# Head of token mixing: tile turns ahead of the angle products, and angle products amid the token products

## The chip, the core and the metric

The kernel runs on one core of one Trainium2 chip. The metric is the device time of one execution in microseconds (us). Shapes are fixed; all inputs and outputs are 32-bit floats. The core has five engines that run at the same time and wait for each other through semaphores: PE (TensorE, matrix products and transposes), DVE (VectorE), ACT (ScalarE), POOL (GpSimd), and SP, which here only issues DMA transfers.

## The reference, cut to what matters

```python
# attention: B=4, H=8, S=768, D=64, 4 sink keys and a window of 128
scores = where(keep, q @ k.T * scale, -1e9);  a = softmax(scores)
x = (a @ v), heads side by side                     # (B, S, 512)

# token mixing
theta = x @ w_theta                                 # (B, S, 512)
zr, zi = x * cos(theta), x * sin(theta)
y = einsum('ts,bsd->btd', w_tok_r, zr) + einsum('ts,bsd->btd', w_tok_i, zi)
u = x + y
x = u + maximum(u @ w_ch, 0)                        # channel mixing

# gated part
gate = sigmoid(causal depthwise conv of x, 5 taps)
out = (gate * (x @ w_val)) @ w_out
```

## The kernel before

The program has three stages, one behind the other on every engine: attention over 16 pairs of heads (a loop written out by hand per engine), token mixing over 4 batches, channel mixing and the gated part over 8 half batches.

Token mixing takes a batch in six tiles of 128 tokens. The fp32 products are made of three passes with a high and a low part of each operand (`split_passes`). For tile s of batch b the work is a chain through all engines:

- `turn` (PE, L1463): four transposes of the tile `x_nat` into the bank `ps_x`.
- `xT` (ACT L1163, L1165; DVE L1295): a raw copy of the turned tile (stored to `xT_scratch` by SP), its high part `xT_hi` and its low part `xT_lo`.
- `theta` (PE, L1474): 12 matmuls of 512 columns into the bank `ps_th`: the angles. There is one bank, so the next `theta` waits for `r_part_done`.
- `turns_out` (DVE L1302, L1305, L1307): rounds the angle to whole turns (`k_big`, `k_int`) and takes them off (`r_part`, which has the place of `k_big`, and in the profile its name). `angle` (DVE L1313, L1317, L1321): `r_raw`, `r_in`, `r_abs`.
- `sines` (ACT L1171, L1173) and `z_parts` (DVE L1330, ACT L1181, POOL L1104): z = x sin and x cos, `z_raw`, with high part `z_hi` and low part `z_lo`.
- `tokens` (PE, L1485): 48 matmuls per tile, into six banks `acc`, one block of banks j = 0 to 5 after the other (6 matmuls of 512 columns each for j < 4, 12 of 256 columns each for j = 4 and 5). At the first tile of a batch each block waits for `u_done`, the addition (DVE L1353, `add_x`) that empties its bank of the batch before.

The loop over tiles (`token_body`) puts on PE at step s: `theta` of the tile two ahead, `turn` of the tile three ahead, then all of `tokens(b, s)`. At the last step of the last batch it puts `first_channels` (PE L1534, channel products) ahead of `tokens`. They wait for `uT_lo` (POOL L1120, `lo_u`), which comes behind the last `z_lo` on POOL, and for the split of the channel weights (`split_w3`: ACT L1192, DVE L1343), which comes behind the last z on ACT and DVE.

The head is the place where attention ends and token mixing begins. There the order is written out by hand on each engine (L368 to L380 for ACT, L454 to L475 for DVE, L581 to L603 for PE), with the last pieces of attention between the first pieces of mixing: `pv` (PE L540, a product with v into `ps_y`), `evac_y` (the copy of `ps_y` into `y_sb`, DVE L409 or ACT L350), `turn_y` (PE L554 and L556, into `ps_o`), and `normalise` (DVE L426, `ps_o` into `x_sb`, counted by `normed`). The banks `acc` lie over those of attention, so PE waits for the last `normalise` before the token products (L602).

Of the kernel before, what the change touches and what calls it, by code (L numbers as in the profile page):

```python
# [21 lines left out]
ACT = mybir.ActivationFunctionType  # L22

P = 128
B, H, S, D = 4, 8, 768, 64
C = H * D
T = S // P
# [4 lines left out]
PAIRS = B * H // 2  # L32
# [22 lines left out]

SyncMix = namedtuple("SyncMix", "begin store_xT run")
PoolMix = namedtuple("PoolMix", "constants chain run")
ScalarMix = namedtuple("ScalarMix", "begin xT sines z_parts run")
VectorMix = namedtuple("VectorMix", "begin xT turns_out angle z_parts run")
TensorMix = namedtuple("TensorMix", "begin turn theta run")  # L60
Mixing = namedtuple("Mixing", "sync gpsimd scalar vector tensor")
# [7 lines left out]
def wait_count(eng, sem, count):  # L69

    if isinstance(count, int) and count <= 0:
        return
    eng.wait_ge(sem, count)
# [21 lines left out]
def fast_path(nc, early, qT, kT, vP, vS, w2, x_scr, xT_scr, uT_scr, w2h, w2l, ident, x_nat, x_in, w3, w3h, w3l, uT0,  # L95
# [6 lines left out]
    IT = PAIRS // 2  # L102
    VISITS = T // 2
# [6 lines left out]
    with ExitStack() as ctx:  # L110
# [37 lines left out]
        y_sb = [place(nc, f"y_sb{m}", [P, 2 * P], F32, U_SB_AT + 8 * P * m) for m in range(VISITS)]  # L148
# [166 lines left out]
        @block.scalar  # L315
        def _(act):
            def exp(n, s, v, t, e):
                g = SCORES * n + 4 * v + 2 * t + e
                k = VISITS * n + v
                i = 2 * v + t  # L320
                lo, hi = columns(i)
                act.wait_ge(maxed, g + 1)
                if t == 0:
                    wait_count(act, turned, 2 * (k - 3) + e + 1)
                    wait_count(act, gathered, 2 * (n - 1) + e + 1)
                nc.scalar.activation(probs[e][:, i, lo:hi], masked[2 * t + e][:, lo:hi], ACT.Exp,  # L326
                                     bias=neg_max[:, s, e, i:i + 1], scale=-1.0,
                                     accum_out=row_sum[:, s, e, i:i + 1]).then_inc(exped, 1)

            def evac(k, m):  # L330

                act.wait_ge(turned, 2 * k + 2)
                wait_count(act, pv_done, k - 2)
                if m > 0:
                    nc.scalar.copy(probsT[1][:, 2 * m:2 * m + 2, :], ps_t[1][:]).then_inc(evac_a, 1)
                else:
                    nc.scalar.copy(probsT[1][:, 0:2, :].rearrange("p t k -> p (t k)")[:, P:4 * P],
                                   ps_t[1][:].rearrange("p t k -> p (t k)")[:, P:4 * P]).then_inc(evac_a, 1)

            def evac_sinks(n):  # L340

                act.wait_ge(turned, 2 * VISITS * (n + 1) + 2)
                wait_count(act, y_turned, VISITS * n)
                nc.scalar.copy(sinkT[:], ps_t[1][:, 0, 0:P]).then_inc(sink_evac, 1)

            def evac_y(n):

                act.wait_ge(pv_done, VISITS * n + 2)
                wait_count(act, y_turned, VISITS * (n - 1) + 2)
                nc.scalar.copy(y_sb[1][:], ps_y[:, 0:2 * P]).then_inc(y_evac[1], 1)  # L350

            def step(it, first=False):
                for s in range(2):
                    n = 2 * it + s
                    for v in range(VISITS):
                        k = VISITS * n + v
                        for t in range(2):
                            for e in range(2):
                                exp(n, s, v, t, e)
                        if v == 1 and not (first and s == 0):  # L360
                            evac_y(n - 1)
                        if not (first and s == 0 and v == 0):
                            evac(k - 1, (v - 1) % VISITS)
                        if v == 1 and not (first and s == 0):
                            evac_sinks(n - 1)

            step(0, first=True)
            with act.Fori(1, IT) as it:  # L368
                step(it)
            mix = mixes.scalar(act)  # L370
            mix.xT(0, 0)
            evac(VISITS * PAIRS - 1, VISITS - 1)
            evac_y(PAIRS - 1)
            evac_sinks(PAIRS - 1)
            mix.xT(0, 1)
            mix.sines(0, 0)
            mix.xT(0, 2)
            mix.z_parts(0, 0)
            mix.sines(0, 1)
            mix.z_parts(0, 1)  # L380
            mix.run()

        @block.vector
        def _(dve):
# [77 lines left out]

            dve.wait_ge(exped, SCORES * PAIRS)
            dve.wait_ge(v_ready, PAIRS)
            mix.turns_out(0, 0)
            evac_y(PAIRS - 1, 2)
            mix.xT(0, 1)
            mix.angle(0, 0)
            normalise(PAIRS - 1, 1, IT - 1, False)
            mix.turns_out(0, 1)  # L470
            mix.xT(0, 2)
            mix.z_parts(0, 0)
            mix.angle(0, 1)
            mix.z_parts(0, 1)
            mix.run()  # L475
# [2 lines left out]
        def _(pe):  # L478
# [112 lines left out]
            turn_y(PAIRS - 1, 1, 0)  # L591
            pe.wait_ge(w_lo_done, B * H)
            pe.wait_ge(maxed, SCORES * PAIRS)
            mix.theta(0, 0)
            mix.turn(0, 1)
            pv(PAIRS - 1, 1, 2, IT)
            turn_y(PAIRS - 1, 1, 1)
            turn_y(PAIRS - 1, 1, 2)
            mix.theta(0, 1)
            mix.turn(0, 2)  # L600

            pe.wait_ge(normed, 2 * PAIRS)  # L602
            mix.run()  # L603
# [217 lines left out]
def mixing(nc, ctx, tag, x_scr, xT_scr, uT_scr, w2h, w2l, ident, x_nat, x_in, w3, w3h, w3l, uT0, conv, out):  # L821
# [336 lines left out]
    def scalar(act):  # L1158
# [104 lines left out]
                    gates(*nxt, 2)  # L1263
                    gates(*nxt, 3)

        def first_sines(b, s):
            act.wait_ge(const2, 1)
            sines(b, s)

        def begin():  # L1270
            xT(0, 0)
            xT(0, 1)
            first_sines(0, 0)
            z_parts(0, 0)
            xT(0, 2)
            chain(0, 1)
# [8 lines left out]
                gates(0, 0, k)  # L1285
            channel_batches(act, channel_body)

        return ScalarMix(begin, xT, first_sines, z_parts, run)

    def vector(dve):  # L1290
        def xT(b, s):
# [165 lines left out]
    def tensor(pe):  # L1457
# [28 lines left out]
                                            stop=s == T - 1 and m == 1 and a == 2, skip_group_check=True)  # L1486
            return last

        def tokens(b, s):

            pe.wait_ge(z_lo_done, 2 * (T * b + s) + 2)
            for j in range(T):
                if s == 0:
                    pe.wait_ge(u_done, T * b + j + 1)
                if j < CB:
                    last = block_of(s, j, acc[j][:], slice(0, C), True)
                else:
                    for h in range(2):
                        last = block_of(s, 2 * (j - CB) + h, acc[j][:, h * (S - C):(h + 1) * (S - C)],
                                        slice(C, S), h == 0)  # L1500

                if s == T - 1:
                    last.then_inc(acc_done, 1)
                elif j == T - 1:
                    last.then_inc(tok_done, 1)

        def token_body(b, last):
            for s in range(T):
                if s < T - 2:
                    theta(b, s + 2)  # L1510
                elif not last:
                    theta(b + 1, s + 2 - T)
                if s < T - 3:
                    turn(b, s + 3)
                elif not last:
                    turn(b + 1, s + 3 - T)
                if last and s == T - 1:
                    first_channels()
                tokens(b, s)

        def first_channels():

# [251 lines left out]
```

## Time and profile before

| | us |
|---|---|
| median of 3 runs | 663.4 (662.34 to 663.86) |
| profiled execution | 665.1 |
| span of its profile | 663.3 |
| attention, up to the head | 0 to about 170 |
| head, up to the first token product | about 170 to 187.7 |
| token mixing | 187.7 to about 470 |
| channel mixing and gate | from 446.9 to the end |

The chain of waits (which work released which, followed back from the last instruction) and the list of waits tell where PE stood. Matmuls are pipelined: a group's start in the timeline can lie a tenth or two before the time at which the chain of waits puts it, and an instruction's own duration (0.39 us for one of 512 columns) is longer than the distance to the next (0.23 us). In the window table a row is: stretch, length, then the busy time of each engine with its count, the granted clock of PE as a share of full speed, the DMA share and GB/s.

### The profile page before, as it was taken

What the parts mean: (1) busy time and instruction counts of PE and PEld (TensorE: products, weight loads), DVE (VectorE), ACT (ScalarE), POOL (GpSimd) and SP (SyncE); (2) the same over time, 40 slices, a digit from 0 to 9 for tenths busy, and PEclk for the clock granted to TensorE, in tenths of its full rate; (3) what the DMA queues carried; (4) which work ended last, traced back from release to release, by engine and by line L of the source; (5) the groups of instructions that cost most, each with busy time, mean ns of one, the idle gap of its engine ahead of it and who ended that gap; (6) DMA issues with size and microseconds to landing.
All of it is one profiled execution on the core that took longest, in us unless ns stands there. A gap on an engine that the chain in (4) does not pass through costs nothing.

```text
span 663.3 us, 14158 instructions
## 1 busy us (share of the span) xinstructions
PE 643.6 (97%) x4016; PEld 549.8 (83%) x4016; DVE 419.3 (63%) x1008; ACT 294.7 (44%) x775; POOL 253.4 (38%) x323
## 2 busy tenths in 40 slices
PE   6899999999889999999999999999999999999995
PEld 4677777777778888888888888889999999999994
DVE  4588788778775446463564547778768458458450
ACT  4777777777542322422232323443243243243231
POOL 4455465565142211313131221346355345345320
PEclk9799999999999999999999999999999999999999
DMA  7376666764512135222432237330520220220011
GB/s 247 132 225 203 240 215 208 243 210 164 176 48 65 33 95 161 60 63 79 133 104 60 82 94 240 103 122 1 190 96 30 67 95 28 69 95 26 23 48 52
DMA packets 61048, 76.70 MB, mean 116 GB/s; under 512 B 4176, under 2 KB 41040, under 8 KB 61008
## 3 DMA queue, kind: packets, MB, share of 16 engines
q1 hardware_dynamic: 61008, 76.24, 35.6%
q8 instruction: 16, 0.26, 0.2%
q14 instruction: 24, 0.20, 0.1%
HBM read 51.06 MB, written 25.17 MB: 115 GB/s over the span
## 4 chain that ended last, share of the span: by engine, by line
PE 92%; issue 2%; POOL 2%; DMA 1%; SPq 1%; DVE 1%; ACT 0%; POOLq 0%; DVEq 0%; ACTq 0%
PE acc L1485 30%; PE ps_p L1534 18%; PE ps_o L1574 10%; PE ps_th L1474 10%; PE ps_s L491 7%; PE ps_t L517 7%; PE ps_y L540 7%; PE ps_o L554 2%; PE ps_x L1463 1%; DMA v_sink<-vS 1%; DMA x_res<-xT_scratch 1%; PE ps_o L556 1%; POOL g_lo L1136 0%; POOL z_lo L1104 0%; SPq L1716 0%
## 5 line engine op out<-in xcount | busy, mean ns | idle before, releaser
L1104 POOL TENSOR_TENSOR z_lo<-z_raw,z_hi 128x512 fp32r<-128x512 f32 x48 | 62.5, 1323 | 206.4 <-ACT z_hi L1181 206.4
L1485 PE MATMUL acc<-w2h,z_hi 128*128 128x512 f32 (+1 forms) x384 | 131.2, 342 | 0.9 <-POOL z_lo L1104 0.9
L1485 PE MATMUL acc<-w2l,z_hi 128*128 128x512 f32 (+1 forms) x384 | 129.3, 337 | 0.0
L1485 PE MATMUL acc<-w2h,z_lo 128*128 128x512 f32 (+1 forms) x384 | 129.3, 337 | 0.0
L326 ACT ACTIVATE probs<-masked,neg_max 128x260 f32<-128x260 f32 (+1 forms) x192 | 92.5, 483 | 37.9 <-DVE neg_max L393 25.5
L393 DVE CUSTOM_DVE_ANT_0 masked<-ps_s,mask 128x260 f32<-128x260 f32 (+1 forms) x192 | 69.0, 403 | 39.1 <-PE ps_s L491 32.5
L1485 PEld LDWEIGHTS acc<-w2h,z_hi 128*128 128x128 f32 x384 | 72.8, 190 | 9.0 <-issue 1.2
L1485 PEld LDWEIGHTS acc<-w2h,z_lo 128*128 128x128 f32 x384 | 72.8, 190 | 8.0
L1485 PEld LDWEIGHTS acc<-w2l,z_hi 128*128 128x128 f32 x384 | 72.9, 190 | 7.8
L1295 DVE TENSOR_TENSOR xT_lo<-ps_x,xT_hi 128x512 fp32r<-128x512 f32 x24 | 16.6, 690 | 78.2 <-ACT xT_hi L1165 78.2
L1398 DVE SCALAR_TENSOR_TENSOR ps_g<-m_raw,conv_w,ps_g 128x384 f32<-128x384 f32 x112 | 62.0, 617 | 0.2
L491 PE MATMUL ps_s<-k_sb,q_sb 64*128 64x260 f32 (+1 forms) x384 | 55.2, 404 | 5.1 <-DMA k_sb<-kT 5.1
L1136 POOL TENSOR_TENSOR g_lo<-g_raw,g_hi 128x384 fp32r<-128x384 f32 x32 | 32.5, 1015 | 71.4 <-ACT g_hi L1237 71.4
L1171 ACT ACTIVATE sin_cos<-r_in 128x512 f32<-128x512 f32 x24 | 15.2, 633 | 97.3 <-DVE r_in L1317 97.3
L517 PE MATMUL ps_t<-ident,probs 128*128 128x128 f32 x352 | 51.5, 283 | 2.1 <-ACT probs L326 2.1
L540 PEld LDWEIGHTS ps_y<-probsT,v_sb 128*64 128x64 f32 x512 | 30.7, 138 | 23.1 <-issue 16.3
L1437 DVE TENSOR_TENSOR g_raw<-ps_p,gate 128x384 f32<-128x384 f32 x32 | 17.8, 557 | 50.7 <-PE ps_p L1534 50.6
L540 PE MATMUL ps_y<-probsT,v_sb 128*64 128x128 f32 (+1 forms) x512 | 49.7, 326 | 0.0
L1128 POOL TENSOR_TENSOR m_lo<-m_raw,m_hi 128x384 fp32r<-128x384 f32 x32 | 33.5, 1046 | 39.8 <-ACT m_hi L1224 39.8
L517 PEld LDWEIGHTS ps_t<-ident,probs 128*128 128x128 f32 x352 | 38.8, 143 | 11.2 <-issue 7.9
L1534 PE MATMUL ps_p<-uT_hi,w_hi 128*128 128x384 f32 x128 | 42.9, 335 | 0.9 <-DVE m_raw L1382 0.9
L491 PEld LDWEIGHTS ps_s<-k_sb,q_sb 64*128 64x128 f32 x384 | 33.1, 194 | 12.9 <-issue 8.4
(93 smaller groups left out, 1435.8 us busy)
## 6 DMA issues: line engine op xcount, KB each, us to landing
k_sb<-kT SPq DMA_DIRECT2D x16, 396.0 KB, 3.9
q_sb<-qT SPq DMA_DIRECT2D x16, 384.0 KB, 3.2
v_sb<-vP SPq DMA_DIRECT2D x16, 384.0 KB, 4.5
x_scratch<-x_sb SPq DMA_DIRECT2D x16, 384.0 KB, 2.6
x_nat<-x_scratch SPq DMA_DIRECT2D x24, 256.0 KB, 3.0
xT_scratch<-xT_raw SPq DMA_DIRECT2D x24, 256.0 KB, 2.2
x_res<-xT_scratch SPq DMA_DIRECT2D x24, 256.0 KB, 3.2
uT_scratch<-u_sb SPq DMA_DIRECT2D x24, 256.0 KB, 2.6
```

The costliest lines, as they stand in the source:

```text
L326: nc.scalar.activation(probs[e][:, i, lo:hi], masked[2 * t + e][:, lo:hi], ACT.Exp, bias=neg_max[:, s, e, i:i + 1], scale=-1.0, accum_out= ...
L393: nc.vector.tensor_tensor_reduce(masked[2 * t + e][:, lo:hi], ps_s[e][t][:, lo:hi], m[:], -SCALE, 3.0e38, ALU.add, ALU.min, neg_max[:, s, ...
L491: nc.tensor.matmul(ps_s[e][t][:, lo:hi], q_sb[s][rows, i * P:(i + 1) * P], k_sb[s][rows, first:first + hi - lo], start=True, stop=True).th ...
L517: last = nc.tensor.transpose(ps_t[e][:, t, side * P:(side + 1) * P], probs[e][:, i, at:at + P], ident[:])
L540: last = nc.tensor.matmul(ps_y[rows, dst:dst + width], v_sb[s][:, j, rows], keysT, start=a == 0, stop=a == len(passes) - 1, skip_group_che ...
L1104: nc.gpsimd.tensor_tensor(z_lo[s % ZR][:, part, :], z_raw[:, part, :], z_hi[s % ZR][:, part, :].bitcast(F32), ALU.subtract).then_inc(z_lo_ ...
L1128: nc.gpsimd.tensor_tensor(m_lo[:, k, :], m_raw[c][:, k, HALO:HALO + L], m_hi[:, k, :].bitcast(F32), ALU.subtract).then_inc(m_lo_done, 1)
L1398: nc.vector.scalar_tensor_tensor(out=summed, in0=src, scalar=w, in1=summed, op0=ALU.mult, op1=ALU.add).then_inc(tap_done[k], 1)
L1474: last = nc.tensor.matmul(ps_th[:], l, r, start=k == 0 and a == 0, stop=k == CB - 1 and a == 2)
L1485: last = nc.tensor.matmul(bank, l, r, start=first and s == 0 and m == 0 and a == 0, stop=s == T - 1 and m == 1 and a == 2, skip_group_chec ...
L1534: last = nc.tensor.matmul(bank[:, 0:L], l, r, start=kk == 0 and a == 0, stop=kk == CB - 1 and a == 2)
L1574: last = nc.tensor.matmul(bank[:], l, r, start=kk == 0 and a == 0, stop=kk == CB - 1 and a == 2)
```

## The change

Four moves, all in order; no product and no transfer is added or dropped, and one small activation is new.

1. PE's head: `turn(0, 1)` now comes ahead of `theta(0, 0)`, and `turn(0, 2)` ahead of `theta(0, 1)`.
2. PE's loop: at each step but a batch's last, blocks 0 to 2 of `tokens` come first, then `theta` and `turn`, then blocks 3 to 5. At the last step all of `tokens` comes behind them, as before.
3. ACT's head: a sine of one column (`sine_table`) brings the sine table in early; the copy `evac_y` of the last `ps_y` moves from DVE to ACT; `xT(0, 2)` comes ahead of the first sines.
4. DVE's head: `xT(0, 1)` ahead of the first rounding, the first angle and z of tile 0 ahead of the second rounding, and the last `normalise` behind the second rounding.

```diff
@@ ScalarE, end of attention
             mix.xT(0, 0)
             evac(VISITS * PAIRS - 1, VISITS - 1)
-            evac_y(PAIRS - 1)
+            evac_y(PAIRS - 1, 1)
             evac_sinks(PAIRS - 1)
             mix.xT(0, 1)
+            mix.sine_table()
+            evac_y(PAIRS - 1, 2)
+            mix.xT(0, 2)
             mix.sines(0, 0)
-            mix.xT(0, 2)
             mix.z_parts(0, 0)
@@ VectorE, end of attention
+            mix.xT(0, 1)
             mix.turns_out(0, 0)
-            evac_y(PAIRS - 1, 2)
-            mix.xT(0, 1)
             mix.angle(0, 0)
-            normalise(PAIRS - 1, 1, IT - 1, False)
-            mix.turns_out(0, 1)
             mix.xT(0, 2)
             mix.z_parts(0, 0)
+            mix.turns_out(0, 1)
+            normalise(PAIRS - 1, 1, IT - 1, False)
             mix.angle(0, 1)
@@ TensorE, end of attention
+            mix.turn(0, 1)
             mix.theta(0, 0)
-            mix.turn(0, 1)
             pv(PAIRS - 1, 1, 2, IT)
             turn_y(PAIRS - 1, 1, 1)
             turn_y(PAIRS - 1, 1, 2)
+            mix.turn(0, 2)
             mix.theta(0, 1)
-            mix.turn(0, 2)
@@ ScalarE, mixing
-        def first_sines(b, s):
+        def sine_table():
+
             act.wait_ge(const2, 1)
-            sines(b, s)
+            nc.scalar.activation(sin_cos[:, 0, 0:1], half_pi[:], ACT.Sin)
@@ TensorE, mixing
-        def tokens(b, s):
-
-            pe.wait_ge(z_lo_done, 2 * (T * b + s) + 2)
-            for j in range(T):
+        def tokens(b, s, banks_of_step):
+
+            if 0 in banks_of_step:
+                pe.wait_ge(z_lo_done, 2 * (T * b + s) + 2)
+            for j in banks_of_step:
@@
         def token_body(b, last):
             for s in range(T):
+
+                ahead_of = 0 if s == T - 1 else T // 2
+                tokens(b, s, range(0, ahead_of))
                 if s < T - 2:
                     theta(b, s + 2)
@@
                 if last and s == T - 1:
                     first_channels()
-                tokens(b, s)
+                tokens(b, s, range(ahead_of, T))
```

How the instructions stand now, at three places. First PE where the head passes into the loop over batches. `ps_th` is a product of `theta`, `ps_x` the four transposes of `turn`; the branch and what is beside it open the loop. Before:

```order
L1474 MATMUL ps_th<-w2l,xT_hi_155 128x512
L1474 MATMUL ps_th<-w2h,xT_lo_157 128x512
L1463 MATMUL ps_x<-ident,x_nat_56 128x128 x4
L951 UNCONDITIONAL_BRANCH
L951 ISA
L73 REGISTER_ALU
L1474 MATMUL ps_th<-w2h,xT_hi_154 128x512
```

and now:

```order
L1477 MATMUL ps_th<-w2l,xT_hi_155 128x512
L1477 MATMUL ps_th<-w2h,xT_lo_157 128x512
L952 UNCONDITIONAL_BRANCH
L952 ISA
L1498 REGISTER_ALU
L1488 MATMUL acc<-w2h,z_hi_158 128x512
L1488 MATMUL acc<-w2l,z_hi_158 128x512
```

The angle product of tile 2 and the turn of tile 3 no longer stand between the head and the first token product.

Second, DVE in the head, from the last `normalise` (`x_sb`) or the angle of tile 0 (`r_abs`) on. Before:

```order
L426 TENSOR_TENSOR x_sb_144<-ps_o,inv_sum 128x512
L1302 TENSOR_SCALAR k_big<-ps_th 128x512
L1305 TENSOR_SCALAR k_int<-k_big 128x512
L1307 SCALAR_TENSOR_TENSOR k_big<-k_int,ps_th 128x512
L1295 TENSOR_TENSOR xT_lo_156<-ps_x,xT_hi_154 128x512
L1330 TENSOR_TENSOR z_raw<-x_nat_54,sin_cos 128x512
L1330 TENSOR_TENSOR z_raw<-x_nat_54,sin_cos 128x512
```

and now:

```order
L1324 SCALAR_TENSOR_TENSOR r_abs<-r_in 128x512
L1298 TENSOR_TENSOR xT_lo_156<-ps_x,xT_hi_154 128x512
L1333 TENSOR_TENSOR z_raw<-x_nat_54,sin_cos 128x512
L1333 TENSOR_TENSOR z_raw<-x_nat_54,sin_cos 128x512
L1305 TENSOR_SCALAR k_big<-ps_th 128x512
L1308 TENSOR_SCALAR k_int<-k_big 128x512
L1310 SCALAR_TENSOR_TENSOR k_big<-k_int,ps_th 128x512
L428 TENSOR_TENSOR x_sb_144<-ps_o,inv_sum 128x512
```

The two products of z stood behind the second rounding and now stand ahead of it; the last `normalise` went from the front of this piece to its end.

Third, PE in the last batch, where the last angle product (`theta` of tile 5) begins. Before, behind the end of the token products of tile 2:

```order
L1485 MATMUL acc<-w2h,z_hi_160 128x256
L1485 MATMUL acc<-w2l,z_hi_160 128x256
L1485 MATMUL acc<-w2h,z_lo_163 128x256
L1474 MATMUL ps_th<-w2h,xT_hi_155 128x512
L1474 MATMUL ps_th<-w2l,xT_hi_155 128x512
```

and now, behind the first three blocks of tile 3:

```order
L1488 MATMUL acc<-w2h,z_hi_158 128x512
L1488 MATMUL acc<-w2l,z_hi_158 128x512
L1488 MATMUL acc<-w2h,z_lo_161 128x512
L1477 MATMUL ps_th<-w2h,xT_hi_155 128x512
L1477 MATMUL ps_th<-w2l,xT_hi_155 128x512
```

It begins 18 token matmuls later than before; the `first_channels` products stand where they stood.

## Rows read from the trace of the kernel before

**Rows 1.** The page: busy time, share and instructions of each engine.

```profile
PE 643.6 (97%) x4016; PEld 549.8 (83%) x4016; DVE 419.3 (63%) x1008; ACT 294.7 (44%) x775; POOL 253.4 (38%) x323
```

**Rows 2.** Who PE waited for, 160 to 250 us: total, times, longest.

```profile
PE ps_th L1474 <- DVE xT_lo L1295: 2.2, 1, 2.2
PE acc L1485 <- POOL z_lo L1104: 0.9, 1, 0.9
```

**Rows 3.** Timeline of the head: start, duration, engine, line, [idle before].

```profile
174.81 0.69 DVE L1302 TENSOR_SCALAR k_big<-ps_th 128x512 f32<-128x512 f32 x1 [2.42 <-PE ps_th L1474]
...
175.04 1.09 PE L540 MATMUL ps_y<-probsT,v_sb 128*64 128x256 f32 x12
175.14 0.59 ACT L1163 COPY xT_raw<-ps_x 128x512 f32<-128x512 f32 x1 [3.11 <-PE ps_x L1463]
...
175.62 0.59 ACT L1165 CAST xT_hi<-ps_x 128x512 fp32r<-128x512 f32 x1
...
176.59 0.42 DVE L409 COPY y_sb<-ps_y 128x256 f32<-128x256 f32 x1
...
177.07 0.33 PE L554 MATMUL ps_o<-ident,y_sb 128*128 128x128 f32 x1 [0.43 <-DVE y_sb L409]
...
178.75 1.28 ACT L1171 ACT_TABLE_LOAD   x1 [2.53 <-DVE r_in L1317]
...
179.31 0.69 DVE L426 TENSOR_TENSOR x_sb<-ps_o,inv_sum 128x512 f32<-128x512 f32 x1
...
183.14 1.28 DVE L1330 TENSOR_TENSOR z_raw<-x_nat,sin_cos 128x512 f32<-128x512 f32 x2
...
183.36 0.49 PE L1474 MATMUL ps_th<-w2h,xT_hi 128*128 128x512 f32 x1 [2.21 <-DVE xT_lo L1295]
...
184.56 3.03 POOL L1104 TENSOR_TENSOR z_lo<-z_raw,z_hi 128x512 fp32r<-128x512 f32 x2 [15.49 <-ACT z_hi L1181]
...
185.06 1.40 DVE L1317 TENSOR_SCALAR r_in<-r_raw 128x512 f32<-128x512 f32 x1
```

**Rows 4.** The chain of waits, head and first steps: start, duration, what.

```profile
171.93 2.76 PE ps_th L1474 x12
...
187.72 8.62 PE acc L1485 x48
...
199.09 0.44 PE ps_x L1463 x4
```

**Rows 5.** Instructions of two tiles: duration ns min/median/max, first and last start.

```profile
L1305 DVE TENSOR_SCALAR k_int<-k_big x24: 426/428/428, 175.5 to 431.0; 128x512 f32<-128x512 f32 x24
...
L1104 POOL TENSOR_TENSOR z_lo<-z_raw,z_hi x48: 1284/1291/1822, 184.6 to 436.7; 128x512 fp32r<-128x512 f32 x48
```

**Rows 6.** Last batch: timeline of DVE and POOL, then the chain of waits.

```profile
430.24 0.69 DVE L1302 TENSOR_SCALAR k_big<-ps_th 128x512 f32<-128x512 f32 x1 [0.55 <-PE ps_th L1474]
...
438.22 5.51 POOL L1120 TENSOR_TENSOR uT_lo<-uT,uT_hi 128x384 fp32r<-128x384 f32 x4
...
446.85 8.32 PE ps_p L1534 x48
```

**Rows 7.** End of batch 0: the chain of waits, then the timeline of DVE.

```profile
245.74 8.38 PE acc L1485 x48
...
247.57 0.68 DVE L1302 TENSOR_SCALAR k_big<-ps_th 128x512 f32<-128x512 f32 x1
...
250.66 0.69 DVE L1321 SCALAR_TENSOR_TENSOR r_abs<-r_in 128x512 f32<-128x512 f32 x1
...
252.78 1.88 DVE L1353 TENSOR_TENSOR u_sb<-acc,x_res 128x512 f32<-128x512 f32 x3
```

**Rows 8.** A stall in attention, then table of stretches (the granted clock follows POOL).

```profile
18.86 0.66 PE L517 MATMUL ps_t<-ident,probs 128*128 128x128 f32 x3 [2.09 <-ACT probs L326]
...
19.00:26.00 7.00, 6.65 (x33) 4.44 (x33) 4.01 (x19) 5.64 (x22) 4.09 (x9) 0.51 0.20 54
180.00:184.00 4.00, 1.79 (x11) 1.29 (x10) 3.19 (x6) 2.39 (x6) 0.00 (x0) 1.00 0.54 164
```

More of the change, by code:

```diff
@@ L57 @@
 PoolMix = namedtuple("PoolMix", "constants chain run")
-ScalarMix = namedtuple("ScalarMix", "begin xT sines z_parts run")
+ScalarMix = namedtuple("ScalarMix", "begin sine_table xT sines z_parts run")
 VectorMix = namedtuple("VectorMix", "begin xT turns_out angle z_parts run")
@@ L344, in evac_sinks, with evac_y @@
                 nc.scalar.copy(sinkT[:], ps_t[1][:, 0, 0:P]).then_inc(sink_evac, 1)
[L346 to L350, printed above, removed]
+            def evac_y(n, m):
+                act.wait_ge(pv_done, VISITS * n + m + 1)
+                wait_count(act, y_turned, VISITS * (n - 1) + m + 1)
+                nc.scalar.copy(y_sb[m][:], ps_y[:, 0:2 * P]).then_inc(y_evac[m], 1)
             def step(it, first=False):
@@ L360, in step @@
                         if v == 1 and not (first and s == 0):
-                            evac_y(n - 1)
+                            evac_y(n - 1, 1)
                         if not (first and s == 0 and v == 0):
@@ L1264, in channel_body @@
                     gates(*nxt, 3)
-        def first_sines(b, s):
+        def sine_table():
             act.wait_ge(const2, 1)
-            sines(b, s)
+            nc.scalar.activation(sin_cos[:, 0, 0:1], half_pi[:], ACT.Sin)
         def begin():
+            sine_table()
             xT(0, 0)
             xT(0, 1)
-            first_sines(0, 0)
+            sines(0, 0)
             z_parts(0, 0)
@@ L1286, in run @@
             channel_batches(act, channel_body)
-        return ScalarMix(begin, xT, first_sines, z_parts, run)
+        return ScalarMix(begin, sine_table, xT, sines, z_parts, run)
     def vector(dve):
```

## The prediction, made before the changed kernel was run

> **What bounds the kernel now.** I read the page's busy times first: PE is busy for 97% of the span [rows 1], so only PE's idle time and its clock can be won or lost. Then the list of PE's waits around the head [rows 2]: 2.2 us before the angle product of tile 2, for `xT_lo`, and 0.9 us before the first token product, for `z_lo`. The timeline adds 0.43 us for the copy `y_sb` on DVE (the row at 177.07 [rows 3]). Together about 3.5 us, and the whole gain of the head cannot exceed that. From 187.72 us on the chain of waits is PE alone, step after step, of which rows 4 show the pieces: there a reordering gives nothing unless it makes PE wait.
>
> **Part 1, the head, walked through.** The question is when the first token product starts. Before, it started at 187.72 with one `theta` (2.75) and one `turn` (0.44) already done [rows 4]. Now these 3.19 us come after it. So the new order breaks even if token products start at 187.72 - 3.19 = 184.53.
> - PE: `turn(0, 1)` takes its 0.44 first, so `theta(0, 0)` starts at 171.93 + 0.44 = 172.37 and ends at 175.13 [rows 4]; `pv` still starts at 175.04 or a tenth later and ends at about 176.15 [rows 3]. DVE's first `k_big` moves from 174.81 to 175.25, as much later as `theta`.
> - ACT: the raw copy and `xT_hi` end 1.1 us behind the turn (turn's end at about 175.1, `xT_hi` at 176.21 [rows 3]), so `xT(0, 1)` ends near 173.5, the table load takes 1.28 [rows 3], the sine of one column an estimated 0.2: done by 175.0, which is before `pv` ends. So the load costs nothing here. If it ran late by more than 1.1 us, it would delay the copy. The copy itself (0.42 on DVE [rows 3], taken as the same on ACT) ends at 176.6 instead of 177.0, since DVE no longer does the rounding first; PE's 0.43 us stall goes.
> - `turn(0, 2)` starts at about 177.2, so `xT_hi` ends near 178.9. DVE has meanwhile run the rounding and the angle of tile 0 without a break. Undisturbed, `r_abs` ends 3.78 us behind the start of `k_big` (250.66 + 0.69 less 247.57 [rows 7]): at 179.0, with `r_in` at 178.3. ACT does the sine (0.63 by an estimate from the copies' 0.59, the cosine a little more) behind `xT_hi`, until 180.1; DVE does `xT_lo` (0.69) in between, and `z_raw` (1.28 [rows 3]) runs from 179.65 to 180.95. Before, it ran from 183.14 [rows 3].
> - POOL started `z_lo` 1.42 us behind the first `z_raw` (184.56 less 183.14 [rows 3]): now at 181.0. Two of them took 3.03 us there while DVE's `r_in` was stretched to 1.40 [rows 3], and take 2 x 1.29 when undisturbed [rows 5]. They end at 183.6 to 184.1.
> - But DVE has `k_big`, `k_int`, `r_part` and the last `normalise` still to do, and PE waits for that too. `k_big` starts at 180.9, `k_int` would start at 181.6, while the first `z_lo` runs. `k_int` was never disturbed before (428 ns at most [rows 5]); `r_in`, the same kind of operation, ended at 186.46, which is 0.6 us behind the end of the first `z_lo` (184.56 + 1.29). I take that: `k_int` ends at 182.9, `r_part` (0.69) at 183.6, `normalise` (0.69 [rows 3]) at 184.25, and the token products start at 184.35.
>
> The Trainium skill, "SBUF — State Buffer", section "SBUF: two separate sides", says that VectorE and GpSimd share one pair of ports as an exclusive lock, which a VectorE operation wants only in a two-port mode or with two inputs in SBUF. By that `k_int` is blocked, and `r_part` and `normalise` with one input in PSUM are not, which is the sum above; without the lock it would be 183.7.
>
> So the head gains 184.53 - 184.35 = 0.2 us; between -0.6 (if `r_part` and `normalise` are held up by the second `z_lo` as well, 0.8 us) and +0.85 (if nothing is). PE's three short stalls become one of 3.6 us. It begins with the end of `theta(0, 1)`: before, PE fell idle at 183.36 - 2.21 = 181.15 [rows 3], behind `theta` and a `turn` of 0.44; now the `turn` is done earlier and the idle time begins at 180.7.
>
> **Part 2, the loop.** At each step but the last, `theta` and `turn` come 18 matmuls of 0.23 us later (12 took 2.75 [rows 4]): 4.1 us. Their consumers follow 4.1 us later. In the middle of a batch nobody is near. From the end of a `theta` to the token products of its tile PE has 0.4 + 4.3 us of its own step and 11.6 of the next one: 16.3. The chain needs 3.8 for the rounding and the angle [rows 7], 4.5 from `z_raw` to the end of `z_lo` (183.14 to 187.59 [rows 3]) and an estimated 2 for the `xT` ahead of it: some 10.5, so 5 us are left.
> - At a batch's end, step 5 keeps its order, but the tokens of the next batch follow at once, without 3.2 us of `theta` and `turn` between. They need `u_sb` of bank 0. It starts at 252.78 and takes 0.69, and ACT's later z delays it by an estimated 0.25: 253.7. PE needs it at 245.74 + 8.38 = 254.12 [rows 7]. The margin is 0.4 us; the next blocks have more. Cost zero, and at most an estimated 0.5 us for each of three batch ends if it is missed.
> - In the last batch the last `theta` is 4.1 us later, so is `k_big` (it waited for just that, 0.55 idle [rows 6]), and all that follows it: z, the weight splits, and on POOL `uT_lo`, which is queued behind the last `z_lo`. It ended at 438.22 + 5.51 = 443.73; it will end at 447.85. PE wants it for `first_channels` at 446.85 [rows 6]. With 0.1 us for the semaphore that is a new stall of 1.1 us, and behind it stand all later products. Bounds: 0.3 to 1.6, from errors of half a microsecond in the shift. The end of the stage hangs on PE's products, so nothing later gives it back.
>
> **Part 3, the clock.** In attention PE stood idle for 2.09 us up to 18.86, and from 19 to 26 us the granted clock was 0.51 in the mean, that is 1.2 GHz instead of 2.4 for about 6.8 of the 7 us [rows 8]. The stall of 2.21 us in the head left the clock at 1.00 (180 to 184 [rows 8]). So a stall of 2 us can do either. The new one of 3.6 us is longer than both. If the clock falls, PE's dense token products run at half speed for as long as it lasts. At 6.8 us that costs 3.4 us; at nothing, 0. What ran in the slow stretch of rows 8 had gaps and small matmuls; the token products are dense, so I take the middle, 1.7 us.
>
> The Trainium skill, "TensorE: Matmul & The Clock Gate", Part 1, names the half rate the default and says that activity releases it. By that rule gathering two short pauses into one long one is what this change should not do; rows 8 show one case for it and one against.
>
> **The sum.** Without the clock: -0.2 + 1.1 = +0.9 us. With it: -0.2 + 1.1 + 1.7 = +2.6 us. On the profiled execution (span 663.3, with 1.8 us around it 665.1) that is 667.7; on the median of 663.4 it is 666.0.
>
> **The rivals.**
> - A, *the clock falls in the head* (forecast), 666.0: for it, the length of the stall; against it, the 2.21 us stall that did nothing.
> - B, *the clock stays*: 663.4 + 0.9 = 664.3, which is no change that can be told. It holds if the pause is not long enough, or if `z_lo` and `normalise` come earlier than I have them.
> - C, *not slower*: `uT_lo` is in time. Its four pieces take 5.51 us [rows 6] while DVE splits weights beside them; in another alignment they may need 4.4, and the stall of 1.1 us is gone. Then -0.2 gives 663.2, and with an undisturbed `k_int` as well -0.85 gives 662.5. The point from which it decides is a `uT_lo` that ends before 446.8.
> - D, *the batch ends*: `u_sb` of bank 0 is later than PE, at three places, by up to 0.5 us each: +0.9 + 1.5 = 665.8, more with the clock. For it: only 0.4 us of margin; against it: the addition of bank 0 waited for nothing but DVE's own chain, which moves with PE.
> - That the change does not do what it says: the order of instructions shows that it does.
>
> **How the numbers follow.** A has 0.46, B 0.30, C 0.12, D 0.12. The forecast is A's 666.0. B and C reach down to 662.5, A with its full price of 3.4 to 667.7. The range of 662.9 to 667.4 leaves out the ends of C and the dearest part of A, some 2 in 10. Less than 0.2% (1.3 us, so 662.1 to 664.7) can hardly be told from no change. Slower by more: most of A (0.38), a quarter of B (0.07), most of D (0.09), together 0.54. Faster by more: only the far end of C and a head better than all my bounds, 0.06. The rest, 0.40, is no change.
>
> **What the changed profile would show.** Right: PE's 0.43 and 2.2 us waits gone, one wait of about 3.6 us before the first `acc` product, put down to `x_sb` or `z_lo`; the table load ahead of the copy of `ps_y` on ACT; `k_int` of tile 1 stretched to over 1 us; a wait of about 1 us of `ps_p` for `uT_lo` near 447; a granted clock of 0.5 behind 184 us for A, 1.00 for B. Wrong: a first token product before 183.5 (the head is worth more than I think), no wait for `uT_lo`, or PE waiting for `u_sb` at the starts of batches.

## The result, and the profile after

The changed kernel takes 666.23 us in the median of 6 executions (664.80 to 667.22), the kernel before 663.05 (661.89 to 664.70, 6 executions). The ratio is 1.0047, with a 95% interval of 1.0028 to 1.0065: 3.2 us slower. The forecast was 666.0. The profiled execution of the changed kernel took 665.62 us, with a span of 663.8.

PE's waits, the longest first (engine, what it waited to do, for what; us in total, times, longest):

```profile
core 0 of [0], span 663.8 us
PE ps_s L492 <- DMA k_sb<-kT: 5.1, 1, 5.1
PE acc L1488 <- DVE x_sb L428: 3.7, 1, 3.7
PE ps_p L1541 <- POOL uT_lo L1121: 1.6, 1, 1.6
PE ps_p L1541 <- DVE m_raw L1385: 1.2, 1, 1.2
```

The waits for `xT_lo` (2.2), `z_lo` (0.9) and `y_sb` (0.4) of before [rows 2, 3] are gone. In their place stand one wait of 3.7 us before the first token product and one of 1.6 us before the first channel product. The head's waits add up to 3.7 now and to 3.5 before, so no time is won there by shorter waits. What can win it is their number: the first matmul behind a wait adds some 0.25 us (below), and there is one such wait now instead of three, which is 0.5 us by an estimate, less the 0.2.

The granted clock behind the long wait (columns: stretch in us, its length, PE's busy time and instructions, granted clock, then DMA):

```profile
178.00:180.00 2.00, 0.00 (x0) 1.00 0.00 0
180.00:182.00 2.00, 0.68 (x2) 0.87 0.03 9
182.00:184.00 2.00, 2.00 (x6) 0.50 1.06 319
184.00:186.00 2.00, 2.00 (x9) 0.78 0.00 0
186.00:188.00 2.00, 2.00 (x10) 1.00 0.00 0
```

PE stands idle from 177.62 to 181.32 at a granted clock of 1.00. The clock falls to the lower of its two levels (0.50, which is 1.2 GHz) just when the products begin, for the last part of the second row, all of the third and the first part of the fourth: (0.13 x 2 + 0.50 x 2 + 0.22 x 2) / 0.5 = 3.4 us in all. The chain of waits shows what that costs (start, us, engine, what it makes, how many):

```profile
169.12 0.44 PE ps_x L1466 x4
169.56 2.79 PE ps_th L1477 x12
176.69 1.28 DVE z_raw L1333 x2
177.97 0.61 DVE k_big L1305
...
181.32 5.96 PE acc L1488 x18
187.28 2.72 PE ps_th L1477 x12
190.00 0.44 PE ps_x L1466 x4
190.44 8.37 PE acc L1488 x48
```

The 18 matmuls that start at 181.32 take 5.96 us. In warm13 below, where the clock stays up, the same 18 take 4.39 us, so the fall costs 1.6 us. (18 x 0.23 = 4.1 leaves out some 0.25 us which the first matmul behind a wait adds in the chain at the full clock too: the first 48 token products of before take 8.62 us [rows 4], the later ones 8.37.)

The last batch, in the chain and in the timeline (the number in brackets is idle time ahead of the instruction):

```profile
432.34 0.69 DVE L1305 TENSOR_SCALAR k_big<-ps_th 128x512 f32<-128x512 f32 x1 [0.23 <-PE ps_th L1477]
437.58 3.09 POOL L1105 TENSOR_TENSOR z_lo<-z_raw,z_hi 128x512 fp32r<-128x512 f32 x2 [6.02 <-ACT z_hi L1182]
440.68 5.66 POOL L1121 TENSOR_TENSOR uT_lo<-uT,uT_hi 128x384 fp32r<-128x384 f32 x4
446.49 0.41 PE L1541 MATMUL ps_p<-uT_hi,w_hi 128*128 128x384 f32 x1 [1.61 <-POOL uT_lo L1121]
```

From `k_big` to the end of `uT_lo` are 14.0 us, against 13.5 before (430.24 to 443.73 [rows 6]).

So the profile after accounts for most of the loss: 1.6 us of clock and 1.6 us of waiting, less what the head wins. In the head, the turn that stands at 169.12 now stands where `theta` stood at 171.93 [rows 4]: this execution reached it 2.81 us sooner. Put back by that, the first token product is at 184.13, and 184.53 would have been even: 0.4 us won. That makes +2.8 us, and the medians say +3.2, with an interval from 1.9 to 4.3.

The two profiled spans differ by 0.5 us only (663.8 and 663.3). The reason is those 2.81 us. In the profile of before the clock was at 0.51 from 19 to 26 us [rows 8], in the profile of after it was 1.00 there, though the change touches nothing in that part. The third group of experiments below is about that.

### The profile page after: what moved, and what is told of

It reads as the page before. It is cut to its first block, busy times and chain, and to the rows that moved or that the text cites. A ratio compares the mean times of both kernels' runs of the same rounds, so it can differ in the third digit from the quotient of the medians.

```text
span 663.8 us, 14161 instructions
## 1 busy us (share of the span) xinstructions
PE 642.4 (97%) x4016; PEld 549.7 (83%) x4016; DVE 417.1 (63%) x1007; ACT 294.8 (44%) x777; POOL 253.8 (38%) x323
## 4 chain that ended last, share of the span: by engine, by line
PE 83%; issue 8%; POOL 4%; DVE 1%; DMA 1%; SPq 1%; ACT 1%; POOLq 0%; ACTq 0%; DVEq 0%
PE acc L1488 24%; PE ps_p L1541 18%; PE ps_o L1581 10%; PE ps_th L1477 8%; PE ps_s L492 6%; PE ps_y L541 6%; PE ps_t L518 6%; PE ps_o L555 2%; POOL z_lo L1105 2%; PE ps_x L1466 1%; POOL uT_lo L1121 1%; DMA x_res<-xT_scratch 1%; DMA v_sink<-vS 1%; PE ps_o L557 1%; ACT probs L326 1%
## 5 line engine op out<-in xcount | busy, mean ns | idle before, releaser
L1164 ACT COPY xT_raw<-ps_x 128x512 f32<-128x512 f32 x24 | 14.1, 585 | 78.7 <-PE ps_x L1466 78.7
```

## The experiments

Ten kernels were run; those of a group ran on one chip beside repeated executions of the kernel before, whose median was 663.13 us (first group, 35 executions), 662.69 (second, 29) and 663.10 (third, 21). The filler products are matmuls whose results nobody reads; all ten compute the full output. The changed kernel's 666.23 us was measured apart from the groups, beside a before of 663.05.

One distance can be read in every trace and leaves out whatever happened before the head: from the start of `turn(0, 0)` to the end of the first 48 channel products. The two rows of the chain of waits that give it, for the changed kernel, and the first of them for before (the second is the row at 446.85 [rows 6]):

```profile
164.97 0.46 PE ps_x L1466 x4
...
446.49 8.56 PE ps_p L1541 x48
...
167.78 0.46 PE ps_x L1463 x4
```

| kernel (one trace each) | distance, us | against before |
|---|---|---|
| before, before_warm8, early10_before | 287.3 to 287.4 | |
| changed kernel | 290.1 | +2.7 |
| last_unsplit | 288.3 | +0.9 |
| warm13 | 288.5 | +1.1 |
| warm13_unsplit | 286.7 | -0.7 |
| head_only | 288.6 | +1.2 |
| head_warm13, early10_head | 287.0 | -0.4 |
| best | 286.3 | -1.1 |
| split_only | 294.0 | +6.6 |

Where the same kernel stretch was traced more than once the distances agree within 0.1 us, while the medians carry intervals of one to two microseconds. So the parts are read here. The clock costs 1.6 us in each of three pairs (290.1 and 288.5, 288.3 and 286.7, 288.6 and 287.0). The late `uT_lo` costs 1.8 in both of its pairs (290.1 and 288.3, 288.5 and 286.7): 1.6 of waiting, and the 48 products behind the wait take 8.56 us instead of 8.32. The new head wins 0.4, and the split of the loop another 0.3 (287.0 and 286.7). Together -0.4 - 0.3 + 1.6 + 1.8 = +2.7.

### First group: each part of the loss alone

**last_unsplit**: the changed kernel, with the loop of the last batch as before.

```diff
-                ahead_of = 0 if s == T - 1 else T // 2
+                ahead_of = 0 if s == T - 1 or last else T // 2
```

> The changed kernel, but in the last batch all token products of a step come behind the angle product and the turn, as before the change. My theory: the wait for uT_lo (1.6 us in the changed profile) goes, nothing else moves, so some 1.1 to 1.6 us less than the changed kernel's 666.2: 664.6 to 665.1. Rival: channel mixing gives the wait back later (its work is bound by VectorE there), and the time stays at 666.2 although the wait is gone.

Measured: 664.36 us (662.78 to 665.63, 11 executions), ratio 1.0011 [1.0000, 1.0022], which is 1.9 us below the changed kernel and a little below the 664.6 to 665.1 expected. PE's waits of this kernel no longer have `uT_lo` among them:

```profile
PE acc L1488 <- DVE x_sb L428: 3.7, 1, 3.7
PE ps_p L1541 <- DVE m_raw L1385: 0.9, 1, 0.9
```

The split of the loop makes `uT_lo` late, and only in the last batch. The rival, that channel mixing gives the wait back, is out.

**warm13**: the changed kernel with 13 filler products on PE in the head's pause.

```diff
             mix.theta(0, 1)
+            for i in range(13):
+                nc.tensor.matmul(ps_s[1][0][:], w2h[:, 0:P], w2h[:, 0:4 * P], start=True, stop=True)
 
             pe.wait_ge(normed, 2 * PAIRS)
```

> The changed kernel with 13 filler matmuls of 512 columns on PE behind the angle product of tile 1 in the head, into a bank that is free; they take 3.0 us and end inside the 3.7 us wait for x_sb. Their products are not used. My theory: the granted clock stays at 1.00 over the head, where the changed profile shows 0.50 from 182 to 184 us; the token products behind it do not run at half speed, and the time falls by some 1.9 us to 664.3. Rival: the clock is no cost (the wait and the later stages make up all of the difference); time 666.2 or more.

Measured: 663.67 us (662.84 to 665.86, 11 executions), ratio 1.0005 [0.9993, 1.0017]; 2.6 us below the changed kernel. The granted clock is 1.00 over the whole head (in this profile it was low from about 19 to 23 us, at the start of attention), and the wait that is left is 0.75 us (timeline and windows):

```profile
178.66 3.11 PE L603 MATMUL ps_s<-w2h 128*128 128x512 f32 x13
182.51 0.49 PE L1490 MATMUL acc<-w2h,z_hi 128*128 128x512 f32 x1 [0.75 <-DVE x_sb L428]
...
182.00:184.00 2.00, 1.49 (x7) 1.00 0.49 150
184.00:186.00 2.00, 2.00 (x10) 1.00 0.62 179
```

From the first product of `theta(0, 1)` to the first token product are 6.71 us here (175.80 to 182.51) and 6.69 in the changed kernel (174.63 to 181.32). So the products neither came earlier nor later: what the fillers change in the head is the clock alone, and that is worth 1.6 us by the traces and 2.6 by the medians (2.4 in the pair of one chip below).

**warm13_unsplit**: both edits.

> Both edits together: filler in the head's wait, and the last batch unsplit. My theory adds them: 666.2 - 1.9 - 1.4 = 662.9, within 0.3 us of the kernel before. What is left is the head's own gain of 0.2 us. If it stays above 664, a third cost is in the loop (the ends of batches).

Measured: 661.97 us (661.40 to 665.05, 11 executions), ratio 0.9985 [0.9971, 0.9998]. It lies 4.3 us below the changed kernel; the two edits alone gave 1.9 and 2.6, together 4.5. On the one chip of this group the pairs are 664.36 and 661.97 (clock: 2.4 us) and 663.67 and 661.97 (`uT_lo`: 1.7 us); the traces say 1.6 and 1.8. With both losses gone the change is a gain: 0.7 us by the trace, about 1 us by the median with an interval from 0.1 to 1.9. The expectation of 662.9 counted 0.2 us for the head and nothing for the split. No third cost is in the loop.

**head_only**: the new head, with every step of the loop as before.

```diff
-                ahead_of = 0 if s == T - 1 else T // 2
+                ahead_of = 0
```

> The change's order of the head on all engines, but the loop over tiles as before (angle product and turn ahead of all token products at every step). PE then runs the angle product of tile 2 as soon as r_part of tile 1 is done: a wait of about 2.9 us, then 3.2 us of work, and z_lo is long done by the first token product. My theory: 0.9 us less idle time than before, 662.1 if the clock stays, 664 if it falls there. Rival: the head's order is worth nothing without the loop's split, 663.1.

Measured: 664.03 us (661.56 to 665.29, 12 executions), ratio 1.0012 [1.0000, 1.0023]. My expectation missed that PE's wait for the last `normalise` stands ahead of the whole loop, so that `theta(0, 2)` waits for `x_sb` as the token products did:

```profile
PE ps_th L1477 <- DVE x_sb L428: 3.7, 1, 3.7
...
182.00:184.00 2.00, 2.00 (x7) 0.52 1.07 323
184.00:186.00 2.00, 2.00 (x8) 0.62 0.00 0
```

The pause is as long as with the split, and the clock falls as well. Here it is `theta` that pays, with 4.61 us for 12 matmuls, where head_warm13 has 3.02 at the same place:

```profile
181.28 4.61 PE ps_th L1477 x12
```

So the 664 expected for a falling clock was met in its size, but not by the wait of 2.9 us that it was built on.

### Second group: what the parts are worth without the losses

**split_only**: the kernel before, with the split loop alone.

```diff
-        def tokens(b, s):
+        def tokens(b, s, banks_of_step):
 
-            pe.wait_ge(z_lo_done, 2 * (T * b + s) + 2)
-            for j in range(T):
+            if 0 in banks_of_step:
+                pe.wait_ge(z_lo_done, 2 * (T * b + s) + 2)
+            for j in banks_of_step:
...
         def token_body(b, last):
             for s in range(T):
+
+                ahead_of = 0 if s == T - 1 else T // 2
+                tokens(b, s, range(0, ahead_of))
                 if s < T - 2:
...
-                tokens(b, s)
+                tokens(b, s, range(ahead_of, T))
```

> The kernel before with the split loop alone; the head's order as before. PE has then nothing to do between the turn of tile 2 (ends 181.15) and the first z_lo (187.6): 6.5 us idle instead of 2.2 + 0.9, and 3.2 us of work come behind it. My theory: +3.2 for the work, +1.5 for uT_lo in the last batch, +1.7 to 3.4 for the clock: 669.5 to 671.2. Rival without a clock effect: 667.8.

Measured: 669.37 us (668.01 to 672.57, 4 executions), ratio 1.0107 [1.0078, 1.0135]. Waits and windows:

```profile
PE acc L1485 <- POOL z_lo L1104: 6.5, 1, 6.5
PE ps_p L1538 <- POOL uT_lo L1120: 1.6, 1, 1.6
...
182.00:184.00 2.00, 0.00 (x0) 0.77 0.00 0
184.00:186.00 2.00, 0.23 (x1) 0.50 0.00 0
186.00:188.00 2.00, 2.00 (x5) 0.50 0.00 0
188.00:190.00 2.00, 2.00 (x6) 0.52 0.00 0
190.00:192.00 2.00, 2.00 (x10) 1.00 0.00 0
```

The loss is 6.7 us. The split needs the new head: with the old one PE runs out of work 6.5 us before z is there. The rival without a clock gave 667.8, which lies below all four executions, if narrowly. The products themselves show the clock's share: they begin at 185.78 and run at half speed until 190, and the first 18 take 6.30 us instead of 4.39, so 1.9 us of the loss.

**head_warm13**: head_only with the 13 filler products.

> The order of the head alone (loop as before), with 13 filler matmuls in its wait. Without the clock's fall the head's order is worth what the idle time says: the wait for x_sb ends at the same place and 3.2 us of angle product and turn come behind it, so 0.2 us better than before: 662.9. The order of the head with filler and the split loop (last batch unsplit) gave 662.0; if the two agree within 0.5 us, the loop's split is worth nothing in itself. Rival: the split gains 0.5 us or more because token products start 3.2 us sooner.

Measured: 661.85 us (661.22 to 663.12, 12 executions), ratio 0.9987 [0.9978, 0.9996]. It is the only kernel here beside warm13_unsplit whose interval lies below 1. The two are equal within 0.2 us in their medians (ratios 0.9987 and 0.9985), as expected; these medians can't tell the split of the loop from nothing. The traces can: 0.3 us, and the angle product amid the token products takes 2.72 us instead of 2.75 at step after step. The gain of the head alone is 0.8 us by the median, with an interval from 0.3 to 1.5, and 0.4 by the trace.

**before_warm8**: the kernel before, with 8 filler products in its wait of 2.2 us for `xT_lo`.

> The kernel before, with 8 filler matmuls (1.9 us) in the 2.2 us wait of its head. My theory: its clock did not fall there in the profile, so filler gives nothing: 663.1, ratio 1.000. Rival: the clock falls there too in some executions, and part of what the filler won in the changed kernel is open to the kernel before: 0.5 to 1 us less.

Measured: 662.61 us (661.62 to 665.08, 12 executions), ratio 0.9998 [0.9984, 1.0012]. The wait is filled (0.3 us left, of 2.2) and the time doesn't move. The distance in the trace doesn't move either (287.3). So in the trace fillers give nothing where the clock didn't fall. Whether the clock falls there in some of the other executions isn't shown: the interval reaches down to 0.9984, as far as the gain of head_warm13, so the medians alone don't rule the rival out.

**best**: warm13_unsplit with 12 fillers, and the last `normalise` on DVE put ahead of the second `turns_out`, so that `k_int` does not meet `z_lo` on POOL.

```diff
             mix.z_parts(0, 0)
-            mix.turns_out(0, 1)
             normalise(PAIRS - 1, 1, IT - 1, False)
+            mix.turns_out(0, 1)
             mix.angle(0, 1)
```

> Filler (12 matmuls) in the head's wait, the last batch unsplit, and the last normalise one place earlier on VectorE: behind z of tile 0, ahead of the second rounding. My theory: normed is then counted about 1.7 us earlier and k_int is pushed behind the first z_lo as before; the first token product waits for z_lo alone and starts 0.3 to 0.5 us earlier than with normalise late. Against the kernel before 661.3 to 661.8 (ratio 0.998). Rival: k_int now collides with the second z_lo and stretches it, and the gain is nothing.

Measured: 662.20 us (660.88 to 663.92, 12 executions), ratio 0.9990 [0.9977, 1.0002]. The trace shows what the edit does:

```profile
178.29 1.28 DVE L1335 TENSOR_TENSOR z_raw<-x_nat,sin_cos 128x512 f32<-128x512 f32 x2
179.50 0.68 DVE L428 TENSOR_TENSOR x_sb<-ps_o,inv_sum 128x512 f32<-128x512 f32 x1
179.71 2.72 POOL L1107 TENSOR_TENSOR z_lo<-z_raw,z_hi 128x512 fp32r<-128x512 f32 x2 [11.83 <-ACT z_hi L1184]
180.81 0.48 DVE L1310 TENSOR_SCALAR k_int<-k_big 128x512 f32<-128x512 f32 x1
...
182.05 0.93 DVE L1318 SCALAR_TENSOR_TENSOR r_raw<-k_int,k_big 128x512 f32<-128x512 f32 x1
182.56 0.49 PE L1490 MATMUL acc<-w2h,z_hi 128*128 128x512 f32 x1 [0.61 <-POOL z_lo L1107]
```

`x_sb` is done early, `k_int` takes 0.48 instead of 1.04, and PE now waits for `z_lo`. What meets `z_lo` now is `r_raw`, with 0.93 us instead of 0.69, and PE doesn't wait for it. From `z_raw` to the first token product are 4.27 us instead of 4.63 (176.69 to 181.32). Those 0.4 us were expected and stand in the distance above (286.3 against 286.7). They can't be told in the median, which missed the 661.3 to 661.8 expected: its interval holds both no gain and a gain of 1.5 us over before. The wait of the head was moved from DVE to POOL, and `z_lo` is as far as this order goes.

### Third group: the fall of the clock at the start of attention

The profile of before has the clock at 0.51 from 19 to 26 us, that of after doesn't, and other kernels lie between. If those 7 us were worth 3 us, a filler there would gain more than the whole change. Both kernels here have ten filler products in PE's pause before 18.86 us:

```diff
+                        if first and s == 1 and v == 1:
+                            pe.wait_ge(w_hi_done, 1)
+                            for i in range(10):
+                                nc.tensor.matmul(ps_o[:, 0:352], w2h[:, 0:P], w2h[:, 0:352], start=True, stop=True)
                         if v > 0:
                             turn(n, v - 1, sinks=v == 1 and started)
```

**early10_head** has them on top of head_warm13:

> The new head's order, the loop of before, 13 filler products in the head, and 10 more filler products (128x352, their results are overwritten unused) on PE at the start of attention, in the pause of 1.5 us up to 18.59 in which PE waits for probs. In the profile of the same kernel without these ten the granted clock was 0.67 from 19 to 22 us and 0.82 from 22 to 26 us, which is half clock for (1 - 0.67) x 3 / 0.5 = 2.0 and 0.18 x 4 / 0.5 = 1.4 us, 3.4 in all. PE is busy there and waits little, so half of it, 1.7 us, is lost. Theory that the early fall comes from that pause and costs its time: the clock stays at 1.00 from 17 to 30 us, the median falls from 661.85 by 1.0 to 1.7 us to 660.2 to 660.9, and the mean granted clock of the span is 0.999. Rival, the start of attention is bound by ACT, DVE and POOL, and a slow PE costs nothing there: the clock is 1.00 and the median stays within 0.4 us of 661.85. Second rival, the pause isn't the cause (much else in that stretch is small and has gaps): the clock falls as before, the median stays.

Measured: 662.96 us (661.93 to 663.43, 11 executions), ratio 0.9994 [0.9985, 1.0003]. It is on another chip than head_warm13, so only the ratios to before can be compared.

**early10_before** has them on top of the kernel before:

> The kernel before with only the 10 filler products at the start of attention, in the pause of 2.09 us up to 18.86. In its profile the granted clock was 0.51 from 19 to 26 us. Theory that the fall comes from the pause and costs time: 1.00 there, and the median falls by 1 to 3 us below that of before (to 660 to 662), with a smaller spread. Rival, nothing is bound by PE there: 1.00 and the same time within 0.4 us. Second rival: the clock falls all the same, and the time stays.

Measured: 662.74 us (662.13 to 663.78, 11 executions), ratio 0.9996 [0.9987, 1.0005]. Its windows:

```profile
17.00:19.00 2.00, 2.00 (x20) 1.00 0.62 227
19.00:22.00 3.00, 2.73 (x21) 1.00 0.04 9
22.00:26.00 4.00, 4.00 (x42) 1.00 0.80 257
```

The clock is up in both, in the profiled executions, and neither median gains over its partner: the ratios to before are 0.9994 against 0.9987 for the one, and 0.9996 for the other. The gain of 1 us or more that was expected lies outside the interval of the second, which ends at 0.9 us.

Yet in the profiled executions the early fall does cost time. The first product behind the pause, in the changed kernel:

```profile
18.50 0.55 PE L518 MATMUL ps_t<-ident,probs 128*128 128x128 f32 x3 [0.83 <-ACT probs L326]
```

From there to the start of `turn(0, 0)` (164.97) are 146.5 us here, where the clock stayed up, and 148.9 in before, where it was low for 6.8 us (18.86 [rows 8] to 167.78). The other traces without early fillers fall in line: 146.0 to 146.4 in the three without a fall (last_unsplit, head_only, warm13_unsplit), 147.6 to 148.1 in the five with a fall of 3.4 us (warm13, head_warm13, before_warm8, split_only, best). So PE's speed is what counts there too, and the fall costs some 1.4 or 2.6 us in an execution that has it. The pause ahead of it was 1.2 to 2.1 us in the six with a fall and at most 0.8 in the four without, which speaks for the pause as its cause but doesn't show it, since the length was not set by an experiment.

The record fits that for before: of its 35 executions in the first group the nine with the highest mean granted clock (0.997 to 0.999) have a median of 662.11 us, the thirteen with the lowest (0.991 to 0.993) 664.08, though it doesn't say where in the span the clock was low. Why the fillers, which keep the clock up in two traces, bring so little at the median stays open.

## Why the prediction was right, point by point

- **The first token product.** Forecast 184.35, measured 184.13 in the time of before (181.32 + 2.81). The steps stand close to their places, each measured one with the same 2.81 added: `xT_hi` ends at 178.80 (forecast 178.9), `z_raw` starts at 179.50 (179.65), `k_int` ends at 182.46 (182.9), `x_sb` ends at 183.78 (184.25). PE then starts 0.35 us behind the end of `x_sb`, where the forecast had 0.1; part of the agreement is that this and the earlier `x_sb` cancel. The head wins 0.4 us in the trace (forecast 0.2), and the same in the distances of head_warm13 and early10_head. The medians of head_warm13 and warm13_unsplit say 0.8 and 1.0, with intervals down to 0.3 and 0.1, which hold the traces' 0.4 and 0.7.
- **The stretched `k_int`.** DVE's timeline has it at 1.04 us beside the first `z_lo`, while `r_part` and `x_sb` keep their 0.69 and 0.68 beside the second:

```profile
178.10 2.67 POOL L1105 TENSOR_TENSOR z_lo<-z_raw,z_hi 128x512 fp32r<-128x512 f32 x2 [11.84 <-ACT z_hi L1182]
178.61 1.04 DVE L1308 TENSOR_SCALAR k_int<-k_big 128x512 f32<-128x512 f32 x1
179.68 0.69 DVE L1310 SCALAR_TENSOR_TENSOR k_big<-k_int,ps_th 128x512 f32<-128x512 f32 x1
180.29 0.68 DVE L428 TENSOR_TENSOR x_sb<-ps_o,inv_sum 128x512 f32<-128x512 f32 x1
```

  This was the choice between 184.35 and 183.7, and it came out on the side taken. The Trainium skill, "SBUF — State Buffer", section "SBUF: two separate sides", describes VectorE's and GpSimd's shared ports as an exclusive lock, which a VectorE operation takes in a two-port mode or with two inputs in SBUF. The trace agrees for `r_part` and `x_sb`, which have an input in PSUM and keep their 0.69 and 0.68 us. `k_int` has a single input, so by that page it would have to run in a two-port mode; the row shows that it was held up, not in which mode it ran.
- **The table load on ACT** costs nothing, as forecast: it starts at 170.69, and `y_sb` at 173.40 waited for PE, not for ACT.

```profile
170.69 1.28 ACT L1270 ACT_TABLE_LOAD   x1
171.98 0.20 ACT L1270 ACTIVATE sin_cos<-half_pi 128x1 f32<-128x1 f32 x1
173.40 0.38 ACT L350 COPY y_sb<-ps_y 128x256 f32<-128x256 f32 x1 [1.22 <-PE ps_y L541]
```

- **The wait for `uT_lo`.** Forecast 1.1 with bounds 0.3 to 1.6, measured 1.6. The mechanism held; the term was too small because the stretch from `k_big` to `uT_lo` grew by 0.5 us (`z_lo` 3.09 us for two instead of 2.55, `uT_lo` 5.66 instead of 5.51). With the 0.2 us that the products behind the wait lose, the price is 1.8. The rival C, a shorter `uT_lo`, was the wrong way round.
- **The clock.** The forecast's middle of 1.7 us between two bounds met 1.6. That was luck in its size: the fall lasted 3.4 us and not 6.8, and dense products at half their rate lose half of it, 1.7 at most, where the forecast had taken half of the span between its bounds. What the argument had right is that the clock falls behind this pause: it did in all three kernels that have 3.7 us of it, and in none of the five where fillers left 0.6 to 0.8. As a rule its comparison of lengths is weak, since the clock also fell after pauses of 1.2 to 1.6 us at the start of attention. Rival B (the clock stays) is out by the windows, and warm13, where only the fillers are added, shows that the clock alone costs this much.
- **The batch ends.** PE waits for `u_sb` at none of them; it has no row among the waits, and rival D is out. The margin of 0.4 us was enough: at the end of batch 0 `u_sb` starts at 251.10 with 0.69 us for its first bank, and PE wants that bank at about 252.4.
- **What the forecast left out.** It had nothing in favour of the split of the loop except the head; the traces give it 0.3 us.
- **The sum.** -0.4 (head) - 0.3 (split) + 1.8 (`uT_lo`) + 1.6 (clock) = +2.7 by the traces, up to the first channel products; forecast -0.2 + 1.1 + 1.7 = +2.6; measured +3.2. The mechanism was right in each loss. That the sums meet within 0.1 us is luck: `uT_lo` was 0.7 too small, head and split together 0.5 too small. The half microsecond up to the median lies behind the first channel products or in the spread: from there to the end of the span the changed kernel has 208.8 us and before 208.1, the twelve traces lie between 207.1 and 208.8, and what sets that isn't shown.

## What to carry to other kernels

Several short waits of PE that are gathered into one long wait are not the same wait: add the granted clock behind it to the sum, and where the wait can't be shortened, a row of matmuls whose results are not used is a cheap try. When a loop's step is reordered for its start, look at its last round too: there the shift meets the next stage with nothing between, and the old order can be kept for that round alone. When medians can't tell half a microsecond, look in the traces for a distance that begins behind everything the change doesn't touch.

## What the runs showed of the hardware

- The clock fell after waits of PE of 3.7 us (three kernels) and 6.5 us (one), and not after waits of 0.6 to 0.8 in the head (five). The length alone doesn't decide: the wait of 2.2 us in the head of before left it alone, while at the start of attention it was low after waits of 1.2 to 2.1 us (six profiles) and not after waits of 0.8 or less (four). After 3.7 us of idleness the granted clock was still 1.00 while PE stood idle and fell as the work began again; so the rows of the wait itself don't show the loss, those behind it do. In split_only it fell within the wait.
- At the lower clock a product of 512 columns came every 0.43 us instead of every 0.23. The fall lasted 3.4 us with dense products in the changed kernel and cost 1.6. In split_only it was back to 1.00 only at about 190, some 4 us after the products had begun, and cost 1.9.
- `k_int` (VectorE) took 1.04 us beside a `z_lo` on GpSimd and 0.43 alone; `r_part` and `x_sb`, with an input in PSUM, kept 0.69 and 0.68 beside it. GpSimd's pair of `z_lo` took 2.67 us there, 2.55 in the last batch of before and 3.09 in that of the changed kernel.
- A fall of the same kind at the start of attention, of 3.4 or 6.8 us, went with a later head by some 1.4 or 2.6 us in the traces. Fillers ahead of it left the median within 0.9 us of before.
- The executions of one kernel spread over 1.5 to 4.6 us (before: 661.13 to 665.54 in the first group). With eleven or twelve executions of a kernel on one chip, a gain of 1 us stood out in two kernels only, and barely.
